# One indirect transfer per step, counts through PSUM, state memsets between steps, the first list ahead of the slots, other fillers

## The chip, the cores and the metric

The kernel runs on one core of one Trainium2 chip. The metric is the device time of one execution in microseconds (us). The engines are TensorE (PE; its weight loads are PEld), VectorE (DVE), ScalarE (ACT), GpSimd (POOL) and SyncE (SP, which issues most DMAs). They run side by side, each in the order of its own program, and meet at semaphores.

## The reference

Three stages follow each other, all in fp32. `moe_` and `moe2_` weights are inputs.

```python
# attention: r, k, v (4, 8, 768, 48), w, u (8, 48)
for t in range(S):
    cur = einsum('bhd,bhe->bhde', u * k_t, v_t)
    y[:, :, t] = einsum('bhd,bhde->bhe', r_t, state + cur)
    state = w * state + einsum('bhd,bhe->bhde', k_t, v_t)
# x = y as 3072 rows of 384
# mixture of 8 experts, one expert for each row
do = x @ w_skip > 0;  logits = x[do] @ w_gate;  e = argmax(logits)
x[do] += softmax(logits)[e] * (relu(x[do] @ w1[e]) @ w2[e])
# dense layer, 384 -> 2048 -> 384
h = x @ w_in;  out = (h * clip(h + 3, 0, 6) / 6) @ w_out
```

## The kernel before

**Attention, 0 to about 143 us.** The 768 positions of each of 4 batches are cut into 6 chunks c of 128; the steps run over chunks outside and batches b inside, 24 steps n = 4c + b. In a step PE makes the scores (`step`, L895) of all heads from the decayed and transposed r and k, transposes r and k of the next step (L830, L839), transposes the last step's result to rows (L849), adds the state's share (L920), the k v products for the new state (L944) and the scores times v (L931). ACT writes the diagonal of the next step's scores into their bank (`diagonal`, L640) and copies kT, xT and rows out. DVE masks the scores into `A_sb` (L1190), scales rT (L1176), updates the state (L1208, L1210) and sums `ruk` over each head into `own` (L1183, `current`), which ACT's diagonal of two steps on needs. POOL forms `k_dec`, `rk` and `ruk` of a step with three products of 128x384 (`step`, L492 to L499). SP loads r, k and v a chunk ahead.

**Routing.** At b = 0 of the next chunk PE makes the logits (L862, some 1 us more); DVE picks the expert at b = 1 and computes where each row goes at b = 2. The running counts by expert, `so_far`, come from one scan over [counts so far, choices]; `carry` (L1249) copies the last column into the first for the next scan. `route_slot` turns ranks into slot numbers, and POOL then scatters (row, weight) pairs to `slot_scratch` in DRAM, one indirect DMA for each batch (`scatters`, L512). The transfers of chunk c - 2 are issued between POOL's steps of chunk c. `carry` writes a choice column and `p_rank` is a constant kept in PSUM.

**Start.** POOL sets its constants, runs step 0, sets the four `state` tiles and the two halves of `nowhere` to their first values (L517 to L519), and runs steps 1 to 3. SP waits for `nowhere` (s_tok, L363) before it writes it over `slot_scratch` (L364), and issues the loads of chunk 1 behind that (L338, L339). PE reads the state of step b only behind s_nought.

**Passage, 143 to 160 us.** The last chunk's slots are computed in two halves. The first expert tile's list is `who`: what `slot_scratch` holds already (`listed`, L1351) plus the rows of the last chunk, summed by PE (`own_slots`, L958). When `who` is there, POOL gathers its rows (`fetch`, L547), 128 and 96 of them. Meanwhile PE does `go_on` transposes of the identity (L965) that nobody reads: ON[0] before the first group of rows is transposed (L992), ON[1] before the second, ON[2] before the first layer. ACT and DVE split the rows in a high and a low part (L721, L1363). DVE has in its queue before that the low parts of w1 (L1297) and the plan of tiles (L1373 to L1387).

**Experts and dense layer, 160 to 710 us.** Tiles of 224 rows, then six blocks of 512 rows; each fp32 product is three products of high and low parts (L980 to L982).

## Time and profile before

| | us |
|---|---|
| median of 3 runs | 712.36 (710.89 to 713.03) |
| profiled execution | 712.37 |
| its span, first to last instruction | 710.60 |
| attention, last v product issued | about 143 |
| first layer of the first tile, first product | 158.93 |

The page gives the busy time and share of each engine and the chain of work that ended last; timelines give each instruction's start, its length, and in brackets the idle time of its engine before it and who ended that. The profiled execution has 1.77 us outside its span.

### The profile page before, as it was taken

How to read it: one execution, taken by the hardware profiler on the slowest of the kernel's cores; microseconds unless marked ns; L12 is line 12 of the kernel's file. 1: busy time of each engine (PE TensorE's matmuls, PEld its weight loads, DVE VectorE, ACT ScalarE, POOL GpSimd, SP SyncE). 2: the span in 40 equal slices, each digit the busy share in tenths (PEclk: the TensorE clock that was granted, in tenths of full speed). 3: DMA queues.
4: the chain of work that ended last, by engine and by line, in shares of the span. 5: the costliest groups of instructions: out<-in, count | busy, mean ns of one | idle time of the engine just before them, and what ended most of it. 6: DMA issues, size and time to landing. Idle time of an engine off the chain costs nothing.

```text
span 710.6 us, 13911 instructions
## 1 busy us (share of the span) xinstructions
PE 697.2 (98%) x5199; PEld 635.1 (89%) x5199; DVE 384.1 (54%) x802; ACT 321.8 (45%) x703; POOL 139.6 (20%) x190
## 2 busy tenths in 40 slices
PE   6999999989999999999999999999999999999998
PEld 4888888879999999889999999999999999998997
DVE  6677667767888888665444334333333343334332
ACT  4777667715555555554433333333333333323222
POOL 8847866532232222100000000000000000000000
PEclk9999999999999999999999999999999999999999
DMA  8788767617666667400011002000200020001001
GB/s 160 160 196 197 178 157 165 228 40 246 226 232 225 213 210 252 122 31 1 0 53 38 0 1 89 1 0 1 90 0 1 1 90 0 1 1 45 1 1 44
DMA packets 106762, 65.71 MB, mean 92 GB/s; under 512 B 79764, under 2 KB 102296, under 8 KB 106704
## 3 DMA queue, kind: packets, MB, share of 16 engines
q1 hardware_dynamic: 102688, 60.13, 29.7%
q0 software_dynamic: 2560, 4.60, 2.0%
q8 instruction: 38, 0.62, 0.4%
q10 hardware_dynamic: 1456, 0.20, 0.2%
q14 instruction: 20, 0.16, 0.1%
HBM read 53.37 MB, written 12.48 MB: 93 GB/s over the span
## 4 chain that ended last, share of the span: by engine, by line
PE 94%; DVE 2%; DMA 1%; POOL 1%; ACT 1%; issue 1%; another core or an unknown queue 0%; DVEq 0%; ACTq 0%; POOLq 0%
PE bank_A L981 8%; PE bank_A L982 8%; PE bank_A L980 8%; PE bank_L L980 4%; PE bank_L L982 4%; PE bank_L L981 4%; PE bank_P L981 4%; PE bank_P L982 4%; PE bank_P L980 4%; PE bank_A L895 4%; PE bank_kT L981 4%; PE bank_kT L982 4%; PE bank_kT L980 3%; PE bank_YT L982 3%; PE bank_YT L981 3%; PE bank_YT L980 3%
## 5 line engine op out<-in xcount | busy, mean ns | idle before, releaser
L1459 DVE TENSOR_TENSOR g_lo<-g,g_hi 128x512 fp32r<-128x512 f32 x96 | 66.4, 692 | 67.1 <-ACT g_hi L769 67.1
L769 ACT ACTIVATE g_hi<-g 128x512 fp32r<-128x512 f32 x96 | 60.7, 632 | 73.1 <-DVE g L1457 73.1
L1457 DVE SCALAR_TENSOR_TENSOR g<-cut,bank_A 128x512 f32<-128x512 f32 x60 | 41.2, 687 | 92.8 <-ACT cut L766 92.8
L766 ACT ACTIVATE cut<-bank_A 128x512 f32<-128x512 f32 x60 | 35.8, 597 | 101.4 <-PE bank_A L982 100.9
L982 PE MATMUL bank_A<-mT_hi,wi_lo 128*128 128x512 f32 x180 | 71.0, 394 | 0.0
L981 PE MATMUL bank_A<-mT_lo,wi_hi 128*128 128x512 f32 x180 | 70.9, 394 | 0.0
L640 ACT ACTIVATE bank_A<-ident,own 128x128 f32<-128x128 f32 x188 | 58.1, 356 | 26.8 <-DVE A_sb L1190 19.7
L980 PE MATMUL bank_A<-mT_hi,wi_hi 128*128 128x512 f32 x180 | 70.0, 389 | 0.0
L1457 DVE SCALAR_TENSOR_TENSOR g<-cut,bank_kT 128x512 f32<-128x512 f32 x36 | 24.7, 687 | 66.6 <-ACT cut L766 66.6
L766 ACT ACTIVATE cut<-bank_kT 128x512 f32<-128x512 f32 x36 | 21.5, 597 | 69.9 <-PE bank_kT L982 69.9
L980 PE MATMUL bank_kT<-mT_hi,wi_hi 128*128 128x512 f32 x108 | 42.1, 390 | 0.9 <-DVE mT_lo L1450 0.9
L982 PE MATMUL bank_kT<-mT_hi,wi_lo 128*128 128x512 f32 x108 | 42.7, 396 | 0.0
L981 PE MATMUL bank_kT<-mT_lo,wi_hi 128*128 128x512 f32 x108 | 42.6, 395 | 0.0
L982 PEld LDWEIGHTS bank_A<-mT_hi,wi_lo 128*128 128x128 f32 x180 | 33.8, 188 | 7.2
L980 PE MATMUL bank_A<-xgT_hi,w_hi 128*128 128x224 f32 x144 | 39.7, 276 | 0.0
L981 PE MATMUL bank_A<-xgT_lo,w_hi 128*128 128x224 f32 x144 | 39.7, 276 | 0.0
L982 PE MATMUL bank_A<-xgT_hi,w_lo 128*128 128x224 f32 x144 | 39.5, 274 | 0.0
L981 PEld LDWEIGHTS bank_A<-mT_lo,wi_hi 128*128 128x128 f32 x180 | 33.8, 188 | 6.0
L980 PEld LDWEIGHTS bank_A<-mT_hi,wi_hi 128*128 128x128 f32 x180 | 33.8, 188 | 5.7
L737 ACT ACTIVATE hT_hi<-bank_A 128x224 fp32r<-128x224 f32 x48 | 17.1, 357 | 44.9 <-PE bank_A L982 42.9
L1417 DVE TENSOR_TENSOR w_lo<-raw,w_hi 128x384 fp32r<-128x384 f32 x64 | 35.7, 558 | 1.3
L1190 DVE TENSOR_TENSOR A_sb<-bank_A,upto 128x512 f32<-128x512 f32 x48 | 30.8, 683 | 7.1 <-PE bank_A L895 6.9
(274 smaller groups left out, 1855.5 us busy)
## 6 DMA issues: line engine op xcount, KB each, us to landing
raw<-in_moe_w_dram SPq DMA_DIRECT2D x24, 512.0 KB
raw<-in_moe_w_dram SPq DMA_DIRECT2D x7, 1536.0 KB
r_in<-in_r_dram SPq DMA_DIRECT2D x24, 192.0 KB, 3.6
v_in<-in_v_dram SPq DMA_DIRECT2D x24, 192.0 KB, 3.4
x_scratch<-y_sb SPq DMA_DIRECT2D x24, 192.0 KB, 2.0
k_in<-in_k_dram SPq DMA_DIRECT2D x23, 192.0 KB, 3.9
m_in<-x_scratch SPq DMA_DIRECT2D x5, 768.0 KB, 5.2
out_dram<-o_sb SPq DMA_DIRECT2D x10, 384.0 KB, 2.8
```

Source lines behind the costliest of these rows:

```text
L640: a = eng.activation(p_A[:, o, q * P:(q + 1) * P], ident[:, :], ACT.Copy, scale=own[n % 2][:, 2 * q + o:2 * q + o + 1])
L737: eng.activation(hT_hi[:, f, :], p_h[f % 3][:, 0:TT], ACT.Relu).then_inc(s_hhi, 1)
L766: eng.activation(cut[f % 2][:, :], p_H[f % 3][:, :], ACT.Relu, bias=0.5, scale=1.0 / 6.0).then_inc(s_cut, 1)
L769: eng.activation(g_hi[f % 4][:, :], g[f % 2][:, :], ACT.Copy).then_inc(s_ghi, 1)
L895: m = eng.matmul(p_A[:, o, q * P:(q + 1) * P], kT[i][half, q, :], rT[i][half, q, :], start=False, stop=True, skip_group_check=True)
L980: eng.matmul(dst, a_hi, b_hi, start=start, stop=False)
L981: eng.matmul(dst, a_hi, b_lo, start=False, stop=False)
L982: return eng.matmul(dst, a_lo, b_hi, start=False, stop=stop)
L1190: eng.tensor_tensor(A_sb[i][:, o, :, :], p_A[:, o, :].rearrange("s (q t) -> s q t", q=NPAIR), mask, ALU.mult).then_inc(s_Aev, 1)
L1417: eng.tensor_tensor(w2_lo[:, f, :], raw2[:, f, :], w2_hi[:, f, :].bitcast(F32), ALU.subtract).then_inc(s_w2lo, 1)
L1457: eng.scalar_tensor_tensor(g[f % 2][:, :], cut[f % 2][:, :], 1.0, p_H[f % 3][:, :], ALU.min, ALU.mult).then_inc(s_g, 1)
L1459: eng.tensor_tensor(g_lo[f % 4][:, :], g[f % 2][:, :], g_hi[f % 4][:, :].bitcast(F32), ALU.subtract).then_inc(s_glo, 1)
```

## The change

Five edits, all in the attention part and the passage:

- `ON` goes from (28, 9, 10) to (40, 9, 5).
- POOL's memset of each `state` tile now stands ahead of the step that follows it, and the last one and the two of `nowhere` behind step 3.
- `scatters` of chunk c - 2: one transfer behind each of the four steps, in place of two behind each of the first two.
- `carry` becomes p_rank x 0 + so_far, an instruction with one operand in PSUM, in place of a copy.
- In the passage `route_slot` of the last half moves behind the two operations that make `who`.

```diff
-ON = (28, 9, 10)
+ON = (40, 9, 5)
...
             step(0, 0, first=True)
-            for t in state:
-                eng.memset(t[:, :, :], 0.0).then_inc(s_nought, 1)
+            for b in range(1, B):
+                eng.memset(state[b - 1][:, :, :], 0.0).then_inc(s_nought, 1)
+                step(b, 0)
+            eng.memset(state[B - 1][:, :, :], 0.0).then_inc(s_nought, 1)
             eng.memset(nowhere[:, :, 0:1], EMPTY).then_inc(s_tok, 1)
             eng.memset(nowhere[:, :, 1:2], 0).then_inc(s_tok, 1)
-            for b in range(1, B):
-                step(b, 0)
             identify(0)
...
                     step(b, c)
-                    if b in (0, 1):
-                        scatters(c - 2, c - 2, range(b * 2, b * 2 + 2))
+                    scatters(c - 2, c - 2, range(b, b + 1))
...
-                eng.tensor_copy(choice[:, :, 0], so_far[:, :, B]).then_inc(s_base, 1)
+                eng.scalar_tensor_tensor(choice[:, :, 0], p_rank, 0.0, so_far[:, :, B], ALU.mult, ALU.add).then_inc(s_base, 1)
...
             route_rank(rts[NC], NC, last, half_B, p_countB)
-            route_slot(rts[NC], last, half_B)
             eng.wait_ge(s_listed, 16)
...
             eng.tensor_tensor(who[0][:, :, 1].bitcast(F32), p_own[:, :, 1], listed[:, :, 1].bitcast(F32), ALU.add).then_inc(s_who0, 1)
+            route_slot(rts[NC], last, half_B)
             split_w1(0, range(1, KC))
```

On POOL at the start, behind step 0, stood this (the numbers behind `ruk`, `state`, `k_dec` and others tell the buffers apart):

```order
L499 TENSOR_TENSOR ruk_84<-rk,u_all 128x384
L517 MEMSET state_90 128x256
L517 MEMSET state_91 128x256
L517 MEMSET state_92 128x256
L517 MEMSET state_93 128x256
L518 MEMSET nowhere 128x256
L519 MEMSET nowhere 128x256
L492 TENSOR_TENSOR k_dec_81<-k_in_77,w_k 128x8x48
```

and now, from step 0 to step 2 and then from step 3 on:

```order
L499 TENSOR_TENSOR ruk_84<-rk,u_all 128x384
L517 MEMSET state_90 128x256
L492 TENSOR_TENSOR k_dec_81<-k_in_77,w_k 128x8x48
L494 TENSOR_TENSOR rk<-r_in_73,k_in_77 128x384
L499 TENSOR_TENSOR ruk_85<-rk,u_all 128x384
L517 MEMSET state_91 128x256
...
L499 TENSOR_TENSOR ruk_85<-rk,u_all 128x384
L519 MEMSET state_93 128x256
L520 MEMSET nowhere 128x256
L521 MEMSET nowhere 128x256
L505 IOTA pairs 128x4
```

Five of the six memsets moved behind step 1, and those of `nowhere` behind step 3.

On POOL in chunk 2, from step 0's last product to step 2's, before:

```order
L499 TENSOR_TENSOR ruk_84<-rk,u_all 128x384
L512 DMA slot_scratch<-pairs,slots 32768x2 x2
L492 TENSOR_TENSOR k_dec_81<-k_in_77,w_k 128x8x48
L494 TENSOR_TENSOR rk<-r_in_73,k_in_77 128x384
L499 TENSOR_TENSOR ruk_85<-rk,u_all 128x384
L512 DMA slot_scratch<-pairs,slots 32768x2 x2
L492 TENSOR_TENSOR k_dec_82<-k_in_78,w_k 128x8x48
```

and now:

```order
L499 TENSOR_TENSOR ruk_84<-rk,u_all 128x384
L512 DMA slot_scratch<-pairs,slots 32768x2
L492 TENSOR_TENSOR k_dec_81<-k_in_77,w_k 128x8x48
L494 TENSOR_TENSOR rk<-r_in_73,k_in_77 128x384
L499 TENSOR_TENSOR ruk_85<-rk,u_all 128x384
L512 DMA slot_scratch<-pairs,slots 32768x2
L492 TENSOR_TENSOR k_dec_82<-k_in_78,w_k 128x8x48
```

Each place holds one transfer, and two more places follow behind steps 2 and 3.

On DVE in the passage, from the rank's last operation to the split of w1, before:

```order
L1282 TENSOR_SCALAR tile_f<-tile_f 128x2
L1286 SCALAR_TENSOR_TENSOR slot_i<-tile_f,slot_f 128x2
L1287 TENSOR_SCALAR slot_p<-slot_i 128x2
L1288 TENSOR_SCALAR slot_c<-slot_i 128x2
L1289 SCALAR_TENSOR_TENSOR slots<-slot_p,slot_c 128x2
L1351 CAST listed_f<-listed 128x2
L1354 TENSOR_TENSOR who<-bank_A,listed_f 128x2
L1355 TENSOR_TENSOR who<-bank_A,listed 128x2
L1297 TENSOR_TENSOR w_lo<-raw_70,w_hi 128x1024 x2
```

and now (line numbers one or two lower):

```order
L1281 TENSOR_SCALAR tile_f<-tile_f 128x2
L1349 CAST listed_f<-listed 128x2
L1352 TENSOR_TENSOR who<-bank_A,listed_f 128x2
L1353 TENSOR_TENSOR who<-bank_A,listed 128x2
L1285 SCALAR_TENSOR_TENSOR slot_i<-tile_f,slot_f 128x2
L1286 TENSOR_SCALAR slot_p<-slot_i 128x2
L1287 TENSOR_SCALAR slot_c<-slot_i 128x2
L1288 SCALAR_TENSOR_TENSOR slots<-slot_p,slot_c 128x2
L1296 TENSOR_TENSOR w_lo<-raw_70,w_hi 128x1024 x2
```

The four slot operations stand behind `who`.

## Rows read from the trace of the kernel before

**Rows 1.** The page: busy time by engine, and the chain that ended last.

```profile
PE 697.2 (98%) x5199; PEld 635.1 (89%) x5199; DVE 384.1 (54%) x802; ACT 321.8 (45%) x703; POOL 139.6 (20%) x190
...
PE 94%; DVE 2%; DMA 1%; POOL 1%; ACT 1%; issue 1%; another core or an unknown queue 0%; DVEq 0%; ACTq 0%; POOLq 0%
```

**Rows 2.** Timeline of POOL, start: start us, us, engine, line, operation, [idle before].

```profile
7.92 1.07 POOL L517 MEMSET state<- 128x256 f32 x4
...
9.48 1.01 POOL L492 TENSOR_TENSOR k_dec<-k_in,w_k 128x384 f32<-128x384 f32 x1
...
11.52 0.99 POOL L499 TENSOR_TENSOR ruk<-rk,u_all 128x384 f32<-128x384 f32 x1
```

**Rows 3.** SP's DMA issues; POOL at step 4; landing of the k loads.

```profile
14.49 0.44 SPq L364 DMA_DIRECT2D slot_scratch<-nowhere  x1
...
15.49 1.81 SPq L339 DMA_DIRECT2D k_in<-in_k_dram  x1
...
19.78 1.00 POOL L492 TENSOR_TENSOR k_dec<-k_in,w_k 128x384 f32<-128x384 f32 x1 [0.54 <-DMA k_in<-in_k_dram]
...
DMA to landing us min/median/max: 3.6/3.8/5.1
```

**Rows 4.** Timelines of DVE and PE, start; the chain at step 4 (start, us).

```profile
7.04 1.43 DVE L1166 TENSOR_TENSOR k_dec<-k_in,w_k 128x192 f32<-128x192 f32 x2 [0.56 <-ACT w_k L625]
...
13.09 1.28 DVE L1190 TENSOR_TENSOR A_sb<-bank_A,upto 128x512 f32<-128x512 f32 x2
...
16.90 1.16 PE L895 MATMUL bank_A<-rT,kT 64*128 64x128 f32 x16 [1.33 <-ACT bank_A L640]
...
32.02 1.12 PE bank_A L895 x16
```

**Rows 5.** The copy of counts (ns min/median/max); DVE and PE timelines.

```profile
L1249 DVE COPY choice<-so_far x6: 162/488/755, 41.0 to 136.7; 128x8 f32<-128x8 f32 x6
...
89.14 1.28 DVE L1190 TENSOR_TENSOR A_sb<-bank_A,upto 128x512 f32<-128x512 f32 x2
...
76.00 1.16 PE L895 MATMUL bank_A<-rT,kT 64*128 64x128 f32 x16 [0.50 <-ACT bank_A L640]
...
98.35 1.16 PE L895 MATMUL bank_A<-rT,kT 64*128 64x128 f32 x16 [0.30 <-ACT bank_A L640]
```

**Rows 6.** Groups by line, POOL, 0 to 160 us: busy, mean ns, idle before.

```profile
L512 POOL DMA_INDIRECT slot_scratch<-pairs,slots x24 | 24.6, 1024 | 40.4 <-DVEq L1290 32.0 <-issue 4.7 <-DMA listed<-slot_scratch 3.5
```

**Rows 7.** Passage to the first tile: timelines of DVE and PE, the chain.

```profile
150.52 0.16 DVE L1354 TENSOR_TENSOR who<-bank_A,listed_f 128x2 int32<-128x2 f32 x1
...
156.16 0.55 DVE L1363 TENSOR_TENSOR xgT_lo<-bank_rT,xgT_hi 128x384 fp32r<-128x384 f32 x1
157.63 0.46 DVE L1363 TENSOR_TENSOR xgT_lo<-bank_kT,xgT_hi 128x288 fp32r<-128x288 f32 x1 [0.92 <-ACT xgT_hi L721]
...
149.77 3.25 PE L965 MATMUL bank_YT<-ident 128*128 128x128 f32 x28
155.00 0.55 PE L992 MATMUL bank_rT<-ident,xg 128*128 128x128 f32 x3 [1.97 <-DMA xg<-x_scratch,who]
...
156.94 2.34 PE L965 MATMUL bank_YT<-ident 128*128 128x128 f32 x10
...
159.69 0.28 PE L980 MATMUL bank_A<-xgT_hi,w_hi 128*128 128x224 f32 x1
...
167.39 0.35 PE L980 MATMUL bank_L<-w_hi,hT_hi 128*128 128x384 f32 x1
...
151.60 3.35 DMA xg<-x_scratch,who
```

**Rows 8.** Windows: length, busy us of each engine, PEclk, DMA share, GB/s.

```profile
150.00:155.00 5.00, 3.03 (x29) 2.79 (x27) 4.57 (x14) 0.00 (x0) 2.79 (x3) 1.00 0.20 54
156.20:156.40 0.20, 0.20 (x3) 0.20 (x2) 0.20 (x2) 0.00 (x0) 0.20 (x1) 0.64 0.00 0
159.60:159.80 0.20, 0.20 (x3) 0.20 (x3) 0.00 (x0) 0.00 (x0) 0.00 (x0) 0.83 1.06 410
```

## The prediction

> **What bounds the kernel now.** I read the page first, then the chain that ended last, then the timelines where TensorE (PE) idles. PE is busy 98% of the span and carries 94% of the chain [rows 1]. So only holes in PE's row, and stretches at the lower clock, can give time back. The dense half has none of either; the change touches the attention part (0 to 143 us) and the passage into the first expert tile (143 to 160 us). Three places matter. First, step 1's scores start after a hole of 1.33 us [rows 4]. Second, in the steps behind a routing step the scores wait 0.50 us (step 12) and 0.30 us (step 16) for ScalarE, which had waited for VectorE (DVE) [rows 5]. Third, behind the 28 filler transposes PE stands still for 1.97 us until the first gathered rows land; at 156.2 to 156.4 the granted clock falls to 0.5 (1.2 GHz) and is back at full speed in 159.6 to 159.8 [rows 7, 8]. I number the steps n = 4c + b.
>
> **State memsets between GpSimd's steps.** Before, six memsets lie between step 0 and step 1 on POOL, 7.92 to 9.48. Now one of about 0.27 us does [rows 2]. Step 1 could start at 8.2, but its k_dec waits for DVE's two first-decay pieces, which end at 7.04 + 1.43 = 8.47 [rows 4]; I take 8.6, so 0.9 earlier than 9.48. The product ruk of step 1 ends at about 11.65 in place of 12.51. DVE's mask of step 0, queued behind the sum over ruk, moves from 13.09 to about 12.2, and the scores of step 1, which come 16.90 - 13.09 = 3.81 later through ScalarE, from 16.90 to 16.0. Taken alone that is 0.9 us; bounds 0.6 (DVE's tiny w_128 product again loses its turn to POOL) and 1.33 (the whole hole).
>
> **What the same move delays.** SyncE waits for the two memsets of `nowhere` (s_tok) before it clears the slot scratch, and behind that clearing stand the r and k loads of chunk 1. Before, they were issued at 14.49 and, for k, 15.49 [rows 3]. Now the `nowhere` memsets come after step 3: 8.6 + 3 x 3.0 + 5 x 0.27 = 18.95 plus the last one's tail, 19.05. So the clearing is issued at 19.1 and k of step 4 at about 20.1, some 4.6 us later. Its landing takes 3.6 to 5.1 us, median 3.8 [rows 3]: 23.9 (23.7 to 25.2). Before, POOL started step 4 at 19.78 after only 0.54 us of waiting [rows 3]; now it idles from 19.8 until 23.9. Its three products end 3.05 us later at 27.0, DVE's sum (0.47 to the next start) lets the mask of step 3 begin at 27.5, and the scores of step 4 follow 3.81 to 3.9 us behind: **31.45**. Before it was 32.02 [rows 4]. Through PE alone, with the 0.9 us gained, it would be 31.1. So the first 32 us give **0.55 us** net; bounds are landing at 25.2 (-0.75) and PE alone (+0.95). I take the median landing, because the queues are nearly empty when it is issued. Later loads catch up: step 5's k lands near 25.7, before POOL has finished step 4.
>
> **One indirect transfer per step.** The 24 transfers keep their number and cost, 1.02 us each [rows 6]. Twenty of them go in groups of one rather than two. After the wait for the slots, step 1 of a chunk starts 1.3 us sooner, which removes waits of DVE for ruk. But those waits lie in steps n = 8, 12, 16, 20, where PE also does the logits (1.0 us more), and the mask is then late by at most 0.75 us. It is hidden there, so I count **0**. The cover for the transfer newly put behind step 3 is POOL's wait for slots, 4.8 us and more per chunk (32.0 us in five waits) [rows 6]. Bounds: -0.2 to +0.3.
>
> **Counts through PSUM.** The six copies of 8 counts take 0.16 us when POOL rests and up to 0.755 us when POOL is in one of its products (median 0.49) [rows 5]. The new form has one operand in PSUM, like its neighbours in the routing, which take 0.17 to 0.22 us; I take 0.18 us. In step 13 the copy is the longest, 0.58 us above the new price. The mask of step 14 (89.14) is late by part of it, DVE's routing work fills step 14 to the brim, and the delay reaches step 16's scores as their hole of 0.30 us [rows 5]: 0.30 back. Step 9's copy is near the median, 0.3 too long, and by the same path about 0.15 of it reaches step 12; I do not expect the rest of that hole of 0.50 us to go, since DVE's lateness there is no larger. Sum **0.45 us**, bounds 0 to 0.8. For these copies the Trainium skill ("SBUF — State Buffer", SBUF: two separate sides) says that a VectorE operation in a two-port mode and a GpSimd operation lock each other out of a shared port for a whole instruction. The trace agrees, 0.16 against 0.755 us.
>
> **First list ahead of slots.** DVE's four slot operations (0.8 us) move behind `who`. It reaches `who` at 149.7 and waits for PE's own-slot sums, which end near 149.95; before, `who` was at 150.52 [rows 7]. So the gather moves from 151.60 to 151.1, and its data (3.35 us behind its start) from 154.95 to 154.45 [rows 7]. Everything behind `who` on DVE is 0.25 us later, since it waits from 149.7 to 149.95. The low parts of the gathered rows, the last thing the first layer needs, were at 156.16 and 157.63. The first now starts at 156.4, and the second is queued right behind it, at 156.87 to 157.35. POOL's last two transfers stay behind the gather and do not wait for the slots.
>
> **Other fillers.** 28 transposes took 3.25 us, 0.116 us each; 40 take 4.64 us and end at 154.4, just as the data land. PE's hole of 1.97 us becomes 0.1 to 0.3. If the clock then stays up, the two row groups and nine fillers end at 154.45 + 0.4 + 1.05 + 0.4 = 156.3, five fillers at 156.9. ScalarE and DVE need about 0.9 us behind the second group (157.2), so DVE's own queue is the limit: first layer at **157.4**. Before, it started behind ten fillers that ran at half clock from 156.94 on, and its fourth product was at 159.69; the next 69 took until 167.39, 0.1116 us each, so that equals a start at 159.36 at full clock [rows 7, 8]. Gain **1.95 us**, bounds 0.7 (clock falls all the same) to 2.15. Behind this point the expert and dense parts are PE's own work and move as a block.
>
> The Trainium skill ("TensorE: Matmul & The Clock Gate", Part 4: PE-mode transpose) says that transposes do not count as busy for the clock. By it the forty would not hold the clock. The rows speak against it: 1.00 all through the pure fillers up to 153.02, and back to 1.00 at 159.6 after a stretch filled mainly with transposes.
>
> **Sum.** 0.55 + 0 + 0.45 + 1.95 = 2.95 us. The profiled run took 712.37 us (span 710.60 and 1.77 around it), the median is 712.36; so 709.4 us. A measurement of this kernel can tell 0.3%, 2.1 us, from no change; below 710.2 counts as faster.
>
> **Rivals.**
> (a) *The clock falls at the same place.* For: PE still has two short holes, and real products are absent from 149.9 to 157.4. Against: the hole ahead of the fall shrinks from 1.97 to 0.3 us. With half clock to 159.6 the first layer starts near 157.6 and loses half of 2 us: transition gain 0.7, time 710.65.
> (b) *Late loads of chunk 1.* Landing after 5.1 us, as the slowest one did, turns +0.55 into -0.75: 710.7. Against: little else is in the queues then.
> (c) *The counts do not escape POOL.* The new instruction waits as the copy did: 0.45 lost, 709.85.
> (d) *Slower: the clock falls inside the forty.* Should a run of pure transposes lose the clock, each further filler costs some 0.22 us in place of 0.116 (the ten at half clock took 2.34 us with the last one's tail [rows 7]). With a fall at 151.0, 29 fillers remain: they end at 157.4, the row groups and nine fillers at 160.9, the first layer starts near 162.0 and runs half as fast for 3 us, like a start at 163.5. That is 4.1 us lost against 159.36, less 1.0 from attention: 715.5. It decides against the change when the fall comes before about 153: 28 fillers are over by then and 12 are not. Against it stands 1.00 in the whole stretch of 28.
>
> **How the numbers follow.** Forecast 709.4: chance 0.50. (a) 0.20, (b) 0.12, (c) 0.11, (d) 0.07. Faster by over 0.3%: forecast and (c), 0.61; within 0.3%: (a) and (b), 0.32; slower: (d), 0.07. The range leaves (d) out. Downward it takes the upper bounds of two terms (0.95, 0.8 in place of 0.55, 0.45: 708.6, and 0.3 for the runs' scatter), upward (a) or (b) with half of the attention gain gone: 708.3 to 711.3.
>
> **What the profile after would show.** Right: step 1's scores at 16.0, a new POOL wait of some 4 us for k before step 4, its scores at 31.4; the count instruction at 0.18 us all six times, no hole before step 16; `who` near 150.0 less the 1 us gained by then; PE without a hole over 0.4 us behind the fillers, clock 1.00 through 156 to 160, first layer some 3 us after the first gathered rows are there. Wrong: scores of step 4 after 32.0, a clock of 0.5 anywhere between the fillers and the first layer, a hole before the first layer longer than 0.7 us, or the gather's rows landing before the forty are done by more than 0.5 us.

## The result, and the profile after

The changed kernel takes **708.17 us** (median of 4 runs, 707.97 to 708.19) where the kernel before, run beside it, takes 712.26 (710.89 to 713.03): ratio 0.9944, interval 0.9927 to 0.9961. The forecast was 709.4 with a range down to 708.3. The direction was right, the gain was 4.1 us instead of 2.95, and the time lies 0.1 us under the range. On a later occasion the same pair gave 706.88 against 709.80, ratio 0.9964 (0.9951 to 0.9978); the forecast's own ratio, 709.4 / 712.37 = 0.9958, lies inside that one and at the upper end of the first.

The page of the changed kernel, part 1 (beside [rows 1]): one per cent more of a shorter span is PE.

```profile
PE 696.0 (99%) x5206; PEld 634.6 (90%) x5206; DVE 381.5 (54%) x802; ACT 321.9 (46%) x703; POOL 140.4 (20%) x190
```

The start, from the timelines of POOL, SyncE's queue and PE (start us, length us, engine, line, operation, [idle before <- what ended it]). These answer to [rows 2 to 4]:

```profile
7.74 0.32 POOL L517 MEMSET state<- 128x256 f32 x1
8.44 1.01 POOL L492 TENSOR_TENSOR k_dec<-k_in,w_k 128x384 f32<-128x384 f32 x1 [0.38 <-DVE k_dec L1165]
...
15.86 1.16 PE L894 MATMUL bank_A<-rT,kT 64*128 64x128 f32 x16 [0.47 <-ACT bank_A L639]
...
19.71 0.73 SPq L339 DMA_DIRECT2D k_in<-in_k_dram  x1
...
23.47 1.00 POOL L492 TENSOR_TENSOR k_dec<-k_in,w_k 128x384 f32<-128x384 f32 x1 [3.99 <-DMA k_in<-in_k_dram]
...
30.93 1.16 PE L894 MATMUL bank_A<-rT,kT 64*128 64x128 f32 x16
```

Only one memset is left between step 0 and step 1; k of chunk 1 is issued over 4 us later and POOL waits 3.99 us for it, yet the scores of step 4 come without a hole. The count instruction and the steps behind the holes of [rows 5] (the first line gives ns, min/median/max):

```profile
L1248 DVE SCALAR_TENSOR_TENSOR choice<-bank_L,so_far x6: 162/163/174, 40.0 to 133.6; 128x8 f32<-128x8 f32 x6
...
74.04 1.16 PE L894 MATMUL bank_A<-rT,kT 64*128 64x128 f32 x16
...
95.65 1.16 PE L894 MATMUL bank_A<-rT,kT 64*128 64x128 f32 x16
```

The passage, beside [rows 7]: timelines of DVE, POOL and PE, and the chain's row for the gather's data.

```profile
146.97 0.16 DVE L1352 TENSOR_TENSOR who<-bank_A,listed_f 128x2 int32<-128x2 f32 x1 [0.32 <-PE bank_A L957]
...
147.89 2.36 DVE L1296 TENSOR_TENSOR w_lo<-raw,w_hi 128x1024 fp32r<-128x1024 f32 x2 [0.16 <-DVE slots L1288]
...
148.05 2.00 POOL L546 DMA_INDIRECT xg<-x_scratch,who  x1 [2.49 <-DVE who L1353]
...
145.91 0.95 PE L957 MATMUL bank_A<-own_rows,in_place 128*128 128x2 f32 x8
146.72 4.57 PE L964 MATMUL bank_YT<-ident 128*128 128x128 f32 x40
152.24 0.55 PE L991 MATMUL bank_rT<-ident,xg 128*128 128x128 f32 x3 [0.96 <-DMA xg<-x_scratch,who]
...
155.11 0.34 PE L979 MATMUL bank_A<-xgT_hi,w_hi 128*128 128x224 f32 x1 [0.54 <-DVE xgT_lo L1362]
...
148.05 3.87 DMA xg<-x_scratch,who
```

PE's hole behind the forty fillers is 0.96 us, where the forecast had 0.1 to 0.3.

Step starts, measured at the first of the sixteen score products, and the marks of the passage, each from one profile:

| us | before | changed | gained so far |
|---|---|---|---|
| scores of step 0 | 10.89 | 10.71 | 0.18 |
| scores of step 4 | 31.98 | 30.93 | 1.05 |
| scores of step 23 | 137.06 | 133.98 | 3.08 |
| last own-slot sums | 148.97 | 145.91 | 3.06 |
| first layer (before: the equal start at full clock) | 159.36 | 155.11 | 4.25 |
| span | 710.60 | 706.4 | 4.2 |

From the first layer to the end of the span every kernel of this study takes 551.2 to 551.4 us; all that follows happens ahead of it. Two questions were open. Why did attention give 3.08 us and not 1.0? And why did the passage, whose PE holes are smaller, give 1.17 and not 1.95?

One fact is needed to read the runs. The mean granted clock of a run is 1.0, or it is 0.990 to 0.998, when the clock was at its lower level (0.5, which is 1.2 GHz) for some us around the passage. In the table, "up" counts the runs at 0.999 or more ("at full clock" in the text), and their median stands beside the median of all. One run of a3 took 1388.08 us; it is left out of the two columns on the right.

| kernel | median | up | median of those |
|---|---|---|---|
| before, in five sets | 711.3, 711.55, 711.76, 709.8, 712.09 | 40 of 113 | 710.03, 710.35, 710.93, 708.4, 710.47 |
| changed (first comparison) | 708.17 | 4 of 4 | 708.17 |
| a1 counts alone | 711.17 | 5 of 10 | 710.33 |
| a2 spread transfers alone | 714.2 | 4 of 10 | 713.0 |
| a3 memsets alone | 710.12 | 5 of 9 | 709.2 |
| a6 slots and fillers | 711.31 | 7 of 10 | 711.05 |
| c1 counts and transfers | 709.94 | 4 of 10 | 708.7 |
| c2 all but the passage | 709.12 | 3 of 10 | 707.8 |
| c3 changed, old fillers | 709.46 | 3 of 10 | 708.0 |
| c4 changed, slots first | 707.79 | 6 of 10 | 707.7 |
| c5 changed, old copy | 712.5 | 8 of 10 | 712.5 |
| b1 plan first | 708.06 | 7 of 8 | 708.06 |
| b2 plan halved | 707.91 | 8 of 10 | 707.9 |
| d1 loads later still | 708.7 | 8 of 10 | 708.6 |
| e1 before, again | 712.87 | 3 of 8 | 710.03 |
| f1 changed, again | 706.88 | 5 of 5 | 706.88 |
| f2 slots first, 46, 9, 9 | 706.81 | 5 of 5 | 706.81 |

a1 to a6 stand beside the first set of before, c1, c2, b1 and d1 beside the second, c3, c4, b2 and e1 beside the third, f1 and f2 beside the fourth, c5 beside the fifth.

### The profile page after: what moved, and what is told of

It is laid out like the page before. It is cut to its first block, busy times and chain, and to the rows that moved or that the text cites. A ratio compares the mean times of both kernels' runs of the same rounds, so it can differ in the third digit from the quotient of the medians.

```text
span 706.4 us, 13934 instructions
## 1 busy us (share of the span) xinstructions
PE 696.0 (99%) x5206; PEld 634.6 (90%) x5206; DVE 381.5 (54%) x802; ACT 321.9 (46%) x703; POOL 140.4 (20%) x190
## 4 chain that ended last, share of the span: by engine, by line
PE 95%; DVE 1%; issue 1%; ACT 1%; POOL 1%; DMA 1%; DVEq 0%; POOLq 0%; ACTq 0%
PE bank_A L980 8%; PE bank_A L981 8%; PE bank_A L979 8%; PE bank_L L979 4%; PE bank_L L981 4%; PE bank_L L980 4%; PE bank_P L980 4%; PE bank_P L981 4%; PE bank_P L979 4%; PE bank_kT L980 4%; PE bank_kT L981 4%; PE bank_kT L979 4%; PE bank_A L894 3%; PE bank_YT L919 3%; PE bank_YT L981 3%; PE bank_YT L980 3%
```

## Attention: the two small parts belong together

**Counts alone (a1)** and **transfers alone (a2)**, each put into the kernel before:

```
a1:  -  eng.tensor_copy(choice[:, :, 0], so_far[:, :, B])
     +  eng.scalar_tensor_tensor(choice[:, :, 0], p_rank, 0.0, so_far[:, :, B], ALU.mult, ALU.add)
a2:  -  if b in (0, 1): scatters(c - 2, c - 2, range(b * 2, b * 2 + 2))
     +  scatters(c - 2, c - 2, range(b, b + 1))
```

> Only the count copy becomes the form with an operand in PSUM. The prediction's theory: all six take 0.16 to 0.18 us, step 15 (to step 16's scores) falls from 5.37 to about 5.05 us, step 11 from 5.57 to about 5.4, the time by 0.45 us. Rival: the stops of PE inside the logits steps 8, 12, 16 and 20 (6.42, 6.49, 6.16, 5.77 us before, 6.01, 6.01, 6.01, 5.54 after the whole change) come from late DVE work behind the copy; then these steps shorten too and the time falls by 1.5 to 2 us. If neither, steps 8 and 12 stay at 6.4 to 6.5.

> Only the indirect transfers are spread, one behind each step. The prediction's theory: 0 us, since the waits for POOL lie under the logits. Rival: the pairs of transfers make POOL late, SyncE issues the next loads at another time, and PE stops inside the logits steps; then steps 8, 12, 16 and 20 fall to 6.01, 6.01, 6.01 and 5.54 us, together 1.3 us, and step 11 (5.57) perhaps by 0.3 to 0.5, while step 15 keeps 5.37.

a1 is level with before: ratio 1.0001 (0.9985 to 1.0016). Steps 11 and 15 take 5.05 us, but steps 8, 12 and 16 stay at 6.36, 6.38 and 6.24, so its rival is out. a2 is **slower**, 1.0037 (1.0021 to 1.0054), some 3 us at full clock, where I had counted 0. A step is counted from its first score product to the next step's. Its steps tell two stories. Steps 8, 12, 16 and 20 took 6.01, 6.01, 6.01 and 5.54 us in place of 6.42, 6.49, 6.16 and 5.77, but steps 14 and 18 took 7.17 in place of 5.39. Where step 14 goes wrong, in the timelines of DVE, POOL and PE of a2:

```profile
83.81 2.57 DVE L1248 COPY choice<-so_far 128x8 f32<-128x8 f32 x1
...
83.24 1.01 POOL L512 DMA_INDIRECT slot_scratch<-pairs,slots  x1 [0.15 <-issue]
...
84.37 1.01 POOL L492 TENSOR_TENSOR k_dec<-k_in,w_k 128x384 f32<-128x384 f32 x1
85.33 1.00 POOL L494 TENSOR_TENSOR rk<-r_in,k_in 128x384 f32<-128x384 f32 x1
...
93.08 1.16 PE L894 MATMUL bank_A<-rT,kT 64*128 64x128 f32 x16 [1.40 <-ACT bank_A L639]
```

A copy of eight numbers for each partition runs from 83.81 to 86.38. It begins 0.57 us into the transfer that now stands at this place on POOL, and ends when the second of the products behind that transfer has ended, at 86.33. Step 18 shows the same: the copy begins 0.57 us into a transfer and takes 2.56 us. A third copy of a2 begins only 0.24 us into a transfer (62.25 against 62.01) and takes 0.16. In the kernel before the worst such wait was 0.755 us [rows 5].

What the spread removes is seen between a1 and the kernel with both parts (c1), here in step 8. First a1 (POOL, DVE, PEld, PE):

```profile
53.61 1.00 POOL L499 TENSOR_TENSOR ruk<-rk,u_all 128x384 f32<-128x384 f32 x1
...
56.30 0.68 DVE L1176 TENSOR_TENSOR rT<-bank_rT,powT_r 128x512 f32<-128x512 f32 x1
...
57.58 0.34 PEld L920 LDWEIGHTS bank_YT<-rT,state 64*64 64x64 f32 x5 [0.25 <-issue]
...
59.56 1.16 PE L895 MATMUL bank_A<-rT,kT 64*128 64x128 f32 x16
```

and c1:

```profile
52.36 1.00 POOL L499 TENSOR_TENSOR ruk<-rk,u_all 128x384 f32<-128x384 f32 x1
...
55.63 0.68 DVE L1175 TENSOR_TENSOR rT<-bank_rT,powT_r 128x512 f32<-128x512 f32 x1
...
59.23 1.16 PE L894 MATMUL bank_A<-rT,kT 64*128 64x128 f32 x16
```

ruk is 1.25 us sooner and DVE's rT product 0.67; the stop of 0.25 us in PE's weight loads, which carried no release that the profile names and so had not caught my eye, is gone, and the next scores follow 0.33 sooner. Whether rT itself or ScalarE's work behind it released that stop is not shown.

**Both together (c1)** and **the changed kernel with the old copy (c5)**, whose only edit is the first diff above, backwards:

> The kernel before with two parts of the change: the counts with an operand in PSUM, and one transfer behind each attention step. Apart, the first took 1.3 us off the start of step 23 (135.76 against 137.06) and the second added 1.9 (138.96), with steps 14 and 18 at 7.17 us. Theory A (the two belong together: the spread transfers bring GpSimd's products level with the count copy, and the copy in SBUF then waits for two of them, 2.57 us; with an operand in PSUM it does not): no step of 7.17 us, steps 8, 12 and 16 at 6.01 us and step 20 at 5.54, steps 11 and 15 at 5.06; step 23 starts 2.0 us sooner than before, near 135.0, and at a mean granted clock of 1.0 the time is 709.0 to 709.6 where the kernel before has 710.0. Theory B (the transfers themselves, or the waits for their slots, hold the steps): steps 14 and 18 stay near 7.17 us, step 23 starts at 138 or later, 712 to 713 us. Theory C, the working of the forecast (spread worth 0): steps 8, 12 and 16 stay at 6.2 to 6.4 us, step 23 at 135.8.

> The changed kernel with the count copy of before, both operands in SBUF, and everything else as changed. In the kernel before, one transfer per step and that copy gave steps 14 and 18 of 7.17 us; with the operand in PSUM they are 5.39 us and steps 8, 12, 16 and 20 keep their 6.01, 6.01, 6.01 and 5.54 us. Theory A (the copy is what fails beside the spread transfers, 2.57 us where it meets two of GpSimd's products): steps 14 and 18 at 7.2 us, 5 at 4 places unchanged, about 4 us more than the changed kernel: ratio to the kernel before about 1.002, 711.5 to 712.5 where that one has 710 to 711. Theory B (with the state memsets moved, the phase between GpSimd and VectorE is another, and the copy falls between two products): at most 1 us more than the changed kernel.

c1 came out as theory A has it: no step of 7.17 us, steps 8, 12, 16 at 6.01, 11 and 15 at 5.06, step 23 at 134.68, ratio 0.9982 (0.9964 to 0.9999), 708.7 us at full clock, 0.3 under what theory A has. c5 is the same from the other side: steps 14 and 18 take 7.16 and 7.18 us, the copy's longest is 2583 ns, and the kernel stands at 712.5, 4.3 us above the changed one's 708.17 of another occasion; beside it the kernel before has a ratio of 1.0009 (0.9991 to 1.0026). From step 0 to step 23 its profile has 127.84 us, the changed kernel's 123.27. So the form of one instruction decides whether the spread transfers gain over a microsecond or lose three. The new form differs from the old in two things, the operation and the place of one operand; which of them frees it was not tried.

**How long is attention before?** At full clock c1 is only 1.3 to 1.6 us under before, though its profile is 2.09 us under the first profile from step 0 to step 23. So I took more profiles of the kernel before:

> The kernel before, unchanged, for another profile. Its runs lie in groups by the mean granted clock: 710.1 at 1.0, 711.3 to 712.7 at 0.998, 712.4 to 714.0 at 0.993. Theory A (one program, whose clock falls or not in the passage): the steps start as in the first profile within 0.3 us (step 23 at 137.1), and the rest differs by the clock behind the fillers; with a mean clock of 1.0 the first layer starts near 157.0 to 157.9. Theory B (the attention part differs from run to run as well): step 23 starts 0.5 us or more from 137.06, with other stops in steps 8 to 20.

> The kernel before, unchanged, for a profile of a run at a mean granted clock of 1.0, which no profile shows so far. At that clock it has 710.0 us where the changed kernel has 708.17, 1.9 us apart, though the steps of the two profiles differ by 2.9 us in attention and the new passage costs 0.3 at equal clock: some 0.8 us are not accounted for. Theory A: in the runs at 1.0 the attention part is 0.8 us shorter than in the first profile (fewer stops in the logits steps), and the shorter part is why the clock stays up. Theory B: attention as before (step 23 at 137.0 to 137.6), the stop of 1.2 us in step 23 is smaller.

> As the run before it: the kernel before once more, with the same two theories; one in three of its runs stands at a mean clock of 1.0.

> As the run before it, a third profile of the kernel before. If all three stand below 1.0, the 0.8 us stay open.

e1 bears out its theory B. From step 0 to step 23 the kernel before takes 126.17 us in the profile that I forecast from, and 127.00 (e1), 125.49 (g1), 125.40 (g2) and 125.30 (g3). g1 and g3 stand at a mean clock of 1.0 (709.88 and 710.37 us), g2 at 0.997 (711.30). Theory A of the last three holds in its first half in two profiles of two: the fully clocked ones have a shorter attention part. That this keeps the clock up does not follow, since g2 is as short and fell. The changed kernel and its relatives with all attention parts and unchanged loads (c2, c3, c4, b1, b2, f1, f2) take 123.2 to 123.5 in each profile. The change takes 2.0 to 3.7 us out of this part and most of its variation. Counts alone (a1, 125.19) differ from g1 to g3 by 0.1 to 0.3 only, and a6, which leaves attention as it was, has 125.49: **the 0.45 us forecast for them was mostly not there**, and the part earns its place as the condition of the spread.

## The start: the late loads are just hidden

**Memsets alone (a3)** and **loads later still (d1)**, the changed kernel with `nowhere` behind seven further small operations of POOL (SyncE's wait on s_tok counts six of them too, 8 in place of 2):

```
a3:  the memset move of the diff, in the kernel before
d1:  eng.memset(state[B - 1]...)
   - eng.memset(nowhere[:, :, 0:1], EMPTY); eng.memset(nowhere[:, :, 1:2], 0)
     identify(0); iota(rank_e), iota(limits), iota(tile_no), iota(so_far), memset(chain_m) x2
   + eng.memset(nowhere[:, :, 0:1], EMPTY); eng.memset(nowhere[:, :, 1:2], 0)
```

> Only the memsets are moved. The prediction's theory: step 0 falls from 6.01 to 5.15 us, the loads of chunk 1 come 4.6 us later, the scores of step 4 begin at 31.45: 0.55 us gained. Rival: the late loads are hidden, step 4 begins at 31.1 and the whole 0.9 us stays. If the stops in the logits steps hang on when things fall against each other and not on the transfers, they change here too.

> The changed kernel with the two memsets of `nowhere` put behind six more small POOL operations (iotas and chain_m), so that SyncE issues the clearing and the loads of chunk 1 some 0.7 us later still. Theory A (k's lateness had just been hidden: the forecast's chain gives 31.0 for a landing at 23.47, PE's own pace 30.93): k lands near 24.2, the scores of step 4 start at 31.6 to 31.7, and 0.6 to 0.7 us stay to the end, 708.8. Theory B (there is room of 0.7 us or more between k's landing and the scores): step 4 starts at 30.9 all the same, 708.2.

a3: ratio 0.9978 (0.9963 to 0.9992), 709.2 at full clock against 710.03, so 0.8 us. Step 0 takes 5.14 us in place of 6.01, and step 4 starts at 31.16, as its rival has it: the late loads are hidden. d1 tells how near the edge this is, in POOL and PE:

```profile
24.02 1.00 POOL L492 TENSOR_TENSOR k_dec<-k_in,w_k 128x384 f32<-128x384 f32 x1 [4.58 <-DMA k_in<-in_k_dram]
...
31.38 1.16 PE L894 MATMUL bank_A<-rT,kT 64*128 64x128 f32 x16 [0.44 <-ACT bank_A L639]
```

From POOL's start to the scores it is 7.36 us. In the changed kernel 23.47 + 7.36 = 30.83, and PE's own pace brings 30.93: had k come 0.10 us later, PE would have waited for it. In d1 k comes 0.55 later, and 0.45 of it shows at step 4 and about 0.4 in the time, 708.6 against 708.17 (on another occasion); I had expected 0.6 to 0.7, since the loads were issued 0.67 later but landed only 0.55 later. Theory A, with less than its price. Step 4 is also late by 0.2 us in c2 (5.19 us for step 3) and in f1 (5.21): there k was issued as early as in the changed kernel (19.74 and 19.61) and POOL started on it at 23.78 and 23.67.

## The passage: an earlier list that brought nothing

**Slots and fillers alone (a6)**, **all but the passage (c2)**, **old fillers (c3)** and **slots first (c4)**, the last three from the changed kernel:

```
a6:  kernel before, ON = (40, 9, 5), route_slot(rts[NC], last, half_B) behind the who operations
c2:  changed kernel, ON = (28, 9, 10), route_slot ahead of s_listed
c3:  changed kernel, ON = (28, 9, 10)
c4:  changed kernel, route_slot ahead of s_listed
```

> Only the passage is changed: slots behind the first list and fillers 40, 9, 5. The prediction's theory: clock 1.00 through the passage, first layer as from 157.4 in place of 159.36, 1.95 us gained. Rival from the trace of the whole change: the gather's first transfer waits for DVE's low part of w1 (POOL 2.00 us in place of 1.22), its data land 0.8 to 1 us later than forecast, and 1.1 us is gained.

> The changed kernel with the passage of the kernel before: slots ahead of the first list, fillers 28, 9 and 10. Attention should run as in the changed kernel (step 23 near 134.0). Theory A (the passage is worth 1.1 us by order and keeps the clock up besides): PE's hole behind the 28 fillers is 1.5 to 2.0 us, the granted clock falls to 0.5 behind it in half of the runs or more, the median is 709.9 to 711.0, and in runs with a mean clock of 1.0 some 709.3. Theory B (attention's 3 us are the whole gain, and its earlier end keeps the clock up too): all runs at a mean clock of 1.0 and a median of 708.2 to 709.0.

> The changed kernel with the fillers of before, 28, 9 and 10; the first list stays ahead of the slots. Reading so far: the earlier `who` gives nothing, since the gather's instruction ends 0.97 us after the first of VectorE's two large products, which starts at the same time in both orders (147.86 and 147.89), and at a mean clock of 1.0 the passage of before is the quicker by 0.3 us (707.8 against 708.2); only the fillers keep the clock up. Theory A (that reading): gather 2.0 us, PE's hole behind the 28 about 2.0 to 2.3 us, runs with a mean clock of 1.0 at 708.0 to 708.2, but half of the runs or more below 0.999 and a median of 709 to 710. Theory B (the order of list and slots keeps the clock up, by bringing the rows sooner): nearly all runs at 1.0, median 708.2, hole 1.2 to 1.5 us.

> The changed kernel with the slots again ahead of the first list; the fillers stay 40, 9 and 5. Theory A (the fillers hold the clock, the order of list and slots costs 0.3 us because VectorE then waits for the own-slot sums with nothing else to do): `who` 0.75 us later, gather 1.22 us and its end unchanged, hole behind the forty 0.7 to 0.95 us, first layer at 154.8 to 154.9 against 155.11, nearly all runs at a mean clock of 1.0, median 707.8 to 707.9, the fastest of all so far. Theory B (the forecast: an earlier `who` brings the rows earlier): rows 0.5 to 0.75 us later than in the changed kernel, median 708.5 or more.

a6 is level with before: ratio 0.9997 (0.9980 to 1.0014), where the forecast's term was 1.95 us. Seven of its ten runs were up, but their median is 711.05, 1.0 us over that of before; 0.3 of it is explained below, the rest is open.

c2 fits neither of its theories: its clock fell in 7 runs of 10, as A has it, but its times are shorter than A's.

Take runs at full clock first. c2, with the old passage, has 707.8; the changed kernel has 708.17; c4, with forty fillers and the old order, 707.7. From the start of the last own-slot sums to the first layer it is 8.90 us in c2, 8.88 in c4 and 8.91 in g1, and 9.20 in the changed kernel, 9.21 in f1; the forecast had 8.43 (157.4 less 148.97). **At equal clock the new order costs 0.3 us.** The rows of g1 (PE):

```profile
147.88 0.95 PE L958 MATMUL bank_A<-own_rows,in_place 128*128 128x2 f32 x8
...
156.79 0.34 PE L980 MATMUL bank_A<-xgT_hi,w_hi 128*128 128x224 f32 x1
```

c4 shows why (DVE, POOL, PE, and its chain's row for the data):

```profile
147.30 2.35 DVE L1296 TENSOR_TENSOR w_lo<-raw,w_hi 128x1024 fp32r<-128x1024 f32 x2
...
148.24 1.22 POOL L546 DMA_INDIRECT xg<-x_scratch,who  x1 [2.98 <-DVE who L1354]
...
145.60 0.95 PE L957 MATMUL bank_A<-own_rows,in_place 128*128 128x2 f32 x8
...
151.62 0.55 PE L991 MATMUL bank_rT<-ident,xg 128*128 128x128 f32 x3 [0.65 <-DMA xg<-x_scratch,who]
...
154.48 0.34 PE L979 MATMUL bank_A<-xgT_hi,w_hi 128*128 128x224 f32 x1 [0.54 <-DVE xgT_lo L1362]
...
148.24 3.04 DMA xg<-x_scratch,who
```

In both kernels the gather's instruction on POOL ends 2.16 us behind the start of DVE's two large products: 147.89 to 150.05 in the changed kernel, 147.30 to 149.46 here. It does so whether it starts 0.16 us or 0.94 us behind them. The first product ends about 1.18 us in, and the instruction ends 0.98 us behind that. Moving `who` forward by 0.5 us lengthened the instruction from 1.22 to 2.00 us and brought its end no sooner. And since DVE stood 0.32 us in front of the own-slot sums with no slots left to fill the time, the large products start 0.28 us later behind these sums (1.98 against 1.70), and the gather's end with them. The step of the forecast that failed in the passage is "So the gather moves from 151.60 to 151.1, and its data (3.35 us behind its start) from 154.95 to 154.45": it added the old 3.35 us, in which 1.22 us of instruction is hidden. The row of the changed kernel has 3.87.

c4 met theory A in its timings (the first layer at 154.48 came even before its 154.8) and was the fastest of its set, but 4 of its 10 runs fell, to 711.4 to 711.6 us; "nearly all runs at 1.0" was wrong. c3 has the gather at 2.01 us and PE's hole at 2.26, falls in 7 runs of 10, and is 708.0 in the others, as theory A has it: **the order of list and slots doesn't keep the clock up**.

**Is it the large product?** b1 puts the twelve operations of the plan ahead of it, b2 seven of them and the rest behind the low parts:

```
b1:  - split_w1(0, range(1, KC))          (behind route_slot)
     + split_w1(0, range(1, KC))          (behind the last operation of the plan)
b2:  as b1, but behind tiles_e .. plan[:, 0:MAXT]; then rows_low(0, t); then the other five
```

> The changed kernel with VectorE's twelve small operations of the expert plan ahead of the two large low-part products of the first weights (1.2 us each), so that GpSimd's first gather no longer meets a large product. Theory A (the gather's instruction waits for the large product that runs when it starts): the gather takes 0.97 to 1.2 us in place of 2.00, its first rows land 0.8 to 1.0 us sooner against `who`, PE's hole behind the forty fillers (0.96) closes, and the first layer then waits for VectorE, whose large products end 6.3 us behind `who`: first layer 0.5 us sooner, 707.5 to 707.9. Theory B (the 2.00 us are the gather's own, or come from the queue): it still takes 2.00 us, the hole stays at 0.9 to 1.0, the time at 708.2 or a little over.

> The changed kernel with VectorE's queue in this order: `who`, slots, first seven operations of the expert plan (1.9 us), the two large low-part products, the low parts of the gathered rows, last five operations of the plan. Theory A (the gather is free of the large products, and VectorE's own queue then sets the first layer): gather 1.0 to 1.1 us, rows at 151.2 or sooner, large products 149.8 to 152.2, low parts of the second group end near 154.0, first layer at 154.0 to 154.3 against 155.11: 707.0 to 707.4. The plan is ready near 155.1 instead of 153.5; if the weight loads that wait for it were on the path, the time would be 0.5 to 1.6 us longer than that. Theory B (ScalarE's copy of the second group waits for VectorE's product as it seemed to when the plan was put first, 153.89 with PE done at 153.06): first layer 154.5 to 154.9, 707.6 to 708.0.

The gather in b1, POOL, PE and DVE:

```profile
147.99 1.07 POOL L546 DMA_INDIRECT xg<-x_scratch,who  x1 [2.48 <-DVE who L1353]
...
151.28 0.55 PE L991 MATMUL bank_rT<-ident,xg 128*128 128x128 f32 x3
...
154.93 0.34 PE L979 MATMUL bank_A<-xgT_hi,w_hi 128*128 128x224 f32 x1 [1.33 <-DVE xgT_lo L1361]
...
153.34 0.55 DVE L1361 TENSOR_TENSOR xgT_lo<-bank_rT,xgT_hi 128x384 fp32r<-128x384 f32 x1
154.33 0.46 DVE L1361 TENSOR_TENSOR xgT_lo<-bank_kT,xgT_hi 128x288 fp32r<-128x288 f32 x1 [0.44 <-ACT xgT_hi L720]
```

1.07 us in place of 2.00 at nearly the same start, and the hole behind the forty closed: the large product held the gather, and that is shown. The time did not follow: 708.06 and 707.91 us, where I expected 707.5 to 707.9 and 707.0 to 707.4. In b1 DVE takes the low parts of the first group at 153.34, as late as in the changed kernel (153.40), and then waits 0.44 us for ScalarE's copy of the second group. That copy starts at 153.89, 0.83 us behind PE's last transpose. In b2 DVE is free from 152.71, but the rows of the second gather land at 152.72 (chain row 149.20 3.52), and ScalarE starts its copy of them at 153.71, 0.47 us behind PE's last transpose; in c4 it starts 0.04 us behind. The time came out as theory B of b2 has it, but its reason, that ScalarE waits for DVE's product, falls, since DVE was idle. What ScalarE waited for, in both, is open.

**What the fillers do.** One and the same kernel has runs in which the clock falls and runs in which it does not; what decides is not shown. e1 and g1 are the same program with the same hole behind the 28 fillers (1.92 and 1.98 us, PE of e1 and of g1):

```profile
155.67 0.86 PE L992 MATMUL bank_rT<-ident,xg 128*128 128x128 f32 x3 [1.92 <-DMA xg<-x_scratch,who]
...
153.93 0.55 PE L992 MATMUL bank_rT<-ident,xg 128*128 128x128 f32 x3 [1.98 <-DMA xg<-x_scratch,who]
```

Windows of e1 (length, busy us of PE, PEld, DVE, ACT, POOL, then PEclk, DMA share, GB/s):

```profile
154.00:156.00 2.00, 0.33 (x2) 0.33 (x3) 1.76 (x8) 0.00 (x0) 1.70 (x2) 0.94 0.46 139
156.00:158.00 2.00, 2.00 (x11) 2.00 (x10) 1.43 (x5) 0.49 (x1) 1.19 (x2) 0.50 0.03 7
```

and of g1:

```profile
152.00:154.00 2.00, 0.07 (x1) 0.07 (x2) 1.76 (x8) 0.00 (x0) 1.64 (x2) 1.00 0.44 123
154.00:156.00 2.00, 2.00 (x20) 2.00 (x21) 1.50 (x6) 0.75 (x2) 1.39 (x2) 1.00 0.07 23
```

With 28 fillers the clock fell in 73 of 113 runs of the kernel before, in 15 of 29 of a1, a2 and a3, in 5 of 8 of e1 and in 20 of 30 of c1, c2 and c3. With 40 or 46 it fell in 3 of 10 of a6 and, in the other kernels (changed, c4, c5, b1, b2, d1, f1, f2), in 11 of 62. Two pairs differ in the fillers alone. From c2 to c4 the median of all goes from 709.12 to 707.79 and that at full clock from 707.8 to 707.7; from c3 to the changed kernel they go from 709.46 to 708.17 and from 708.0 to 708.17. So the fillers are worth 1.3 us in the median and cost at most 0.2 at full clock, and the 0.3 us above belong to the order of list and slots. These pairs span two occasions each, and in a6, with the attention of before, no gain in the median was seen.

A fall can cost more now. In the sets of before it costs up to 3.7 us over the median at full clock; with forty fillers 1.3 and 1.9 in d1, 3.6 in b1, 3.7 to 3.9 in c4, 1.5 and 5.1 in b2, 3.5 and 5.2 in c5. c5's profile is one of the fallen, 717.72 us:

```profile
145.00:146.00 1.00, 0.73 (x7) 0.49 (x5) 0.90 (x7) 0.60 (x1) 0.00 (x0) 1.00 0.00 0
146.00:147.00 1.00, 1.00 (x11) 1.00 (x11) 0.40 (x4) 0.00 (x0) 0.00 (x0) 0.95 0.07 2
147.00:148.00 1.00, 1.00 (x8) 1.00 (x7) 0.83 (x6) 0.59 (x2) 0.35 (x1) 0.50 0.00 0
...
154.50 7.51 PE L964 MATMUL bank_YT<-ident 128*128 128x128 f32 x40
```

Here it falls at 146.9, ahead of the forty, and these take 7.51 us in place of 4.57. a6's profile (713.87 us) has the same, with 6.28 us for the forty, and so had a3 and g2 a fall at 144 to 150 with 28 fillers (g2: 0.61 over 146 to 150).

> The changed kernel, unchanged, for more runs beside the kernel before. The first comparison had four runs, all at a mean granted clock of 1.0. Theory A (the forty fillers keep the clock up as a rule, and it is the ordering that decides by chance in the rest): 8 runs in 10 or more at a mean clock of 0.999 or above, median 708.1 to 708.3, a few at 709.5 to 712. Theory B (four runs were luck, and the fall comes as often as with 28 fillers, 7 runs in 10): median 709.5 or more. In both the attention part has the same length as in the first profile (step 23 at 133.8 to 134.0).

> The changed kernel with the slots ahead of the first list and 46, 9 and 9 fillers. With 40, 9 and 5 and this order the median was 707.79, but 4 runs of 10 stood at a mean clock of 0.992 or 0.993 and 711.4 to 711.6; PE had holes of 0.65 us behind the forty and 0.54 us ahead of the first layer. Six more transposes take 0.68 us, four more 0.46 us. Theory A (the holes in the passage are what lets the clock fall): both holes under 0.15 us, nearly all runs at 0.999 or above, first layer at 154.5 to 154.6, median 707.6 to 707.8. Theory B (the fall has another origin, such as the stretch before the passage): 3 to 5 runs in 10 at 0.993 as before. Theory C (rows and transposes now collide): first layer 0.2 us later or more, 708.0.

f1: five runs, all up, 706.83 to 707.13; theory A of it as to the clock, with a time 1.2 us under its 708.1. f2, with both holes closed as far as the fillers reach (0.17 us behind the forty-six, none ahead of the first layer, which starts 9.07 us behind the own-slot sums), is level with it, 706.81 (706.67 to 706.96), all five up. Since f1 never fell either, that set can't tell whether the holes let the clock fall; it stays open. Beside them the kernel before fell in 7 runs of 9. Neither f2 nor c4 beats the changed kernel by an amount that is more than a tenth of a per cent.

## Why the prediction was wrong, step by step

The sum was made against the first profile, and in its terms the misses are:

| term | forecast | measured | by |
|---|---|---|---|
| start | 0.55 | 1.05 | step 4 at 30.93, forecast 31.45 |
| transfers | 0 | 2.03 | together with the counts |
| counts | 0.45 | (in the line above) | a1's attention 0.1 to 1.8 shorter, by the profile of before |
| passage | 1.95 | 1.17 | first layer against step 23 |
| sum | 2.95 | 4.25 | |

**State memsets.** Right in mechanism and size: 0.86 us at step 1 (forecast 0.9), confirmed by a3 and by c1 against c2 (708.7 to 707.8). 0.18 us of the 1.05 is the first step's own start, which varies from 10.53 to 10.98 between profiles.

**Late loads.** Right in mechanism, mis-sized by 0.5: k was issued at 19.71 and not 20.1, POOL started at 23.47 and not 23.9, and the way to the scores is 7.36 us and not 7.55. Rival (b) had the right place, but not its size: d1 shows that k could come only 0.1 us later before it costs time, and no run had the landing of 5.1 us that (b) prices.

**One transfer per step.** The step that failed most, and the one that put the time under the range: 2.03 us together with the counts, where the sum had 0 and 0.45 and the lower end of the range 0 and 0.8. "But those waits lie in steps n = 8, 12, 16, 20, where PE also does the logits (1.0 us more), and the mask is then late by at most 0.75 us. It is hidden there, so I count **0**." The wait was not hidden: what stands behind the mask reached PE, as far as known through DVE's rT product or ScalarE's work behind it. The four steps were 0.41, 0.48, 0.15 and 0.23 us longer than they need be, and steps 11 and 15, whose holes the forecast gave to the counts, 0.51 and 0.32. The first part was to be read in the first profile by laying the four logits steps beside each other. The bound of -0.2 was wrong on the other side: alone the part costs 3 us.

**Counts through PSUM.** The price, 0.163 us six times, was right (forecast 0.18), and rival (c) is out. The share of the path was not: by the sum's method it should have paid alone. A copy waits while POOL works, by 0.6 us in the kernel before and by 2.4 us in a2. The Trainium skill ("SBUF — State Buffer", SBUF: two separate sides) has the loser of the shared port blocked for the whole instruction of the other; the trace agrees that it waits, but a2's 2.57 us outlasts a whole product of POOL and more. I had looked at the six copies as they lay before, not as the spread would lay them. The gather's 2.00 us and b1's 1.07 show a wait the other way round, POOL's instruction held by a large DVE product; the forecast moved the gather along DVE's queue without looking at what DVE ran beside it.

**First list ahead of slots.** Against the own-slot sums `who` came 0.49 us earlier (forecast 0.5); the 0.5 us for the data were not there. **Fillers.** 0.114 us each, forecast 0.116; the clock stayed up in the first comparison, though PE's hole behind them was 0.96 us. But the forecast took the fall in the profile of before as the state of that kernel, when 40 of its 113 runs don't have it, and its gain of 1.95 us is against a fallen run. Rival (a) held the right idea the wrong way: the fall is an event of single runs and not of a place. Rival (d), a slow stretch of fillers at half clock, exists: the profiles of c5 and a6 have it, though the clock falls ahead of the forty and not inside them. It cost 3.5 and 5.2 us in c5's two fallen runs, against the 6.1 between its 715.5 and the forecast. Whether the 4 fallen runs of c4 are of this kind no profile shows. It never came in the nine runs of the changed kernel itself.

So the adding of parts hid one that is no sum (the spread is worth something only with the new form of the counts) and two things that vary from run to run in the kernel before: its attention part and its clock. That the total came within 1.3 us was luck in part: 1.6 us too little for attention's transfers and counts and 0.5 for the start, 0.8 too much for the passage. At full clock the change is 1.5 us beside its own set (706.88 against 708.39) and 1.9 to 2.8 against the other sets' medians (708.17 against 710.03 to 710.93). In the pair of profiles 1.48 us of the 4.25 are the fall in the kernel before (10.39 us from own-slot sums to first layer, against 8.91 in g1), less the 0.3 of the order, and 0.7 to 0.9 are attention longer than in g1 to g3.

## What to carry to other kernels

When a change moves work on one engine, lay its long instructions beside the short ones of the engine that shares its memory with it, in the new order: a tiny copy took 2.57 us and a gather's instruction 2.00 us because of what ran beside them, and the form with an operand in PSUM was the cure for the first. Take several profiles before you size a term from holes of 0.3 us: the kernel before varied by 1.7 us in its attention part. And where a median sits between two clock levels, count the runs at each level; the fillers bought 1.3 us in the median here, in kernels with the new attention, and next to nothing in a run that would not have fallen.

## What the runs showed of the chip

- A DVE copy of 128x8 between two places in SBUF lasted 2.57 and 2.58 us (a2, c5), across the rest of a POOL transfer and two POOL products of 1.0 us, in place of 0.16. It had begun 0.57 us into the transfer; one that began 0.24 us into a transfer took 0.16.
- A POOL gather instruction lasted 2.00 us beside DVE's two-operand products of 1.2 us, and 1.07 us beside small ones.
- Forty transposes in a row ran at a granted clock of 1.00 throughout (changed kernel, 146.72 to 151.29); in a6 the clock came back from 0.50 to 1.00 while PE did little but transposes (151.72 to 158.00).
- The same hole of 1.9 to 2.0 us in PE let the clock fall in one run and not in the next. Falls also came at 144 to 147 us, with PE at transposes and small products (c5: PE busy 0.73 and 1.00 of the two us up to the fall; g2: PE busy through all of 144 to 146, where the mean clock is 0.92).
- In step 23 PE stops between its last products of scores times v (ended by "issue") or takes 1.5 us for sixteen of them in place of 1.08, while DVE waits 0.73 to 1.54 us for a "remote" release. In f1 and f2 both are absent, and f1's span is 705.3 us against 706.4 for the same program before. What it is, was not tried.
